# Earlier weight loads and splits, and half as many clears of twice the size, in a hashed-attention and MoE kernel

## The chip, the cores and the metric

The kernel runs on one core of one Trainium2 chip. The metric is the device time of one execution in microseconds. Before the change it is 832.31 us, the median of three runs (830.89 to 832.5).

## The reference

The inputs are q, k, v of shape (2, 8, 768, 64): 16 heads of 768 tokens. Each head's attention is masked by a hash: tokens attend to one another only if the signs of six projections agree. The result feeds a mixture of 8 experts (one expert per token, capacity 384), and that a dense layer pair.

```python
q_bits = (np.einsum('bhsd,dk->bhsk', q, proj) > 0)        # six bits, likewise for k
mask = q_bucket[:, :, :, None] == k_bucket[:, :, None, :]
scores = np.where(mask, scale * np.matmul(q, k.transpose(0, 1, 3, 2)), -1e9)
attn = softmax(scores);  x = attn @ v                      # rows of (1536, 512)
disp[e, counts[e]] = x[i]        # expert e = argmax of x @ w_gate, at most 384 rows each
y = relu(disp @ w1) @ w2;  out[i] = gate_w[i] * y[e, pos[i]]
h = out @ w_in;  result = (h * clip(h + 3, 0, 6) / 6) @ w_out
```

All products are made in two parts: a number is split into a high part, rounded to the matmul's format, and a low part, the rest. That holds for the weights too, hence the splits of weights spoken of below.

## The kernel before

The program has one instruction stream for each engine, written out by hand, with waits on semaphores between them. An engine takes its instructions in order. It has three stages: attention over the 16 heads (to about 325 us), routing and the 8 experts (to about 550 us), and the dense pair.

A head is named (turn, side), number 2*turn+side; tiles that alternate between heads have one copy a side. `LAST` is (7, 1). While TensorE works on head h, it also prepares h.next() (transposes of q and k at L1168, hash products at L1177) and multiplies the probabilities of h.prev() by v (L1246 to L1248).

One head in its steps, and where they stand:
- SP loads q and k (`load_qk`, L372) and v (`load_v`, L380) from memory.
- TensorE turns q and k; ScalarE writes the high part to q_ext (`high_qk`, L709), VectorE the low part to qk_lo (`low_qk`, L900).
- SP moves halves of these tiles between partitions by DMA (`place_head`, whose five moves are all at L384): k_ext<-q_ext, k_pair<-q_ext, k_pair<-qk_lo, then qk_lo<-q_ext, then k_ext<-q_ext (the hash bits). The first waits for `high_qk`. The fourth waits until the third has landed.
- VectorE makes the hash bits from the hash product (`bits`, L906). `bits` waits for the first two moves to have landed, since it writes over the same tile.
- TensorE makes the scores a first time, tile by tile (`max_tile`, L1191), VectorE takes their row maxima (`take_max`, L911, six a head) and negates them (`minus_max`, L916 to L919). In VectorE's order of a head, the `bits` of the next head stand between the fourth and the fifth `take_max`.
- TensorE turns the maxima (`turn_max`, L1205), ScalarE copies them (L713), and TensorE makes the scores a second time, as `cross` (L1220) and `direct` (L1228); ScalarE takes the exponential of each of the six tiles (L720) and its high part (L724), VectorE and GpSimd take low parts (L937, L614).

Beside the heads, three kinds of work for the expert stage are spread over the attention stage:
- The weights of expert 0, 4 MB in four loads (`load_part`, L406): two go out between `place_head(0,1)` and `load_v(1,0)`, two between `place_head(1,0)` and `load_v(1,1)`. ScalarE waits for all four before head (1,0), and then takes the high part of one eighth of them (`high_parts`, L734) in every head (turn, 0) from turn 1 on, with two in a row before `LAST`. GpSimd takes the low parts (`first_low`, L604) in heads (turn, 1), one before its work on `LAST`, one after it.
- The clears: the buffers x_slots and y_rows in memory are set to a row of zeros, in `CLEARS` = 12 pieces, each two DMAs (L430, L432), one piece a head, between `place_head(h)` and the `load_v` of the next. Before it scatters rows, GpSimd waits for `32 * CLEARS` on the clears' semaphore.
- At the end of the stage the first loads for expert 1 follow.

All loads, moves and clears of this stage are issued from SP, on one queue of the 16 DMA engines.

Of the kernel before, what the change touches and what calls it, by code (L numbers as in the profile page):

```python
# [19 lines left out]
def hashed_attention_moe_kernel(nc, q, k, v, proj, w_gate, w1, w2, w_in, w_out, out, capacity):  # L20
    B, H, S, D = q.shape
    NBITS = proj.shape[1]
    HEADS = B * H
# [37 lines left out]
    LOADS = 4  # L61
    LC = WC // LOADS
    CHUNKS = 8
    CC = WC // CHUNKS
    HB = 4
    CLEARS = HEADS - 4
    assert SLOTS // P % CLEARS == 0 and NT % CLEARS == 0
    assert WC == DC * F2 == FC2 * DM and ST > MT
    GT = BANK
# [19 lines left out]
    with ctx:  # L89
# [128 lines left out]
        def sem(name):  # L218
            return ctx.enter_context(nc.semaphore(name))
# [56 lines left out]
        raw_in = [sem(f"raw_in{i}") for i in range(LOADS)]  # L276
# [66 lines left out]
        def lo_use(h, first=False):  # L343

            return h.i * 3 + (1 if first else 0)

        def hash_use(h, first=False):

            return lo_use(h, first) + 1

        LAST = Head((HEADS - 1) // 2, 1)
# [11 lines left out]
        def _(sp):  # L363
# [3 lines left out]
            def load_qk(h, first=False):  # L367
                if not first:

                    sp.wait_ge(prep_full, h.i * 3 - 5)  # L370
                for part, source in enumerate((q_v, k_v)):
                    sp.dma_start(qk_raw[:, h.side, :, part * D:part * D + D],  # L372
                                 source[h.i, :, :].rearrange("p (c d) -> p c d", d=D)).then_inc(qk_in[h.side], 16)

            def load_v(h, first=False):
                if not first:

                    sp.wait_ge(v_lo_done, h.i - 1)
                    sp.wait_ge(v_summed, h.i - 1)
                sp.dma_start(v_raw[:, h.side, :, :].rearrange("p c d -> p (c d)"), v_v[h.i, :, :]).then_inc(v_in[h.side], 16)  # L380

            def move(to, of):

                return sp.dma_start(to.bitcast(F32), of.bitcast(F32))  # L384

            def place_head(h, first=False):
                sp.wait_ge(qk_hi_done, h.i + 1)
                move(k_ext[h.side][0:D, :], q_ext[h.side][D:2 * D, :]).then_inc(k_hi_placed, 16)
                move(k_pair[h.side][0:D, :], q_ext[h.side][D:2 * D, :]).then_inc(k_hi_placed, 16)

                sp.wait_ge(prep_free, lo_use(h, first))
                move(k_pair[h.side][D:2 * D, :], qk_lo[h.side][D:2 * D, :]).then_inc(k_lo_placed, 16)

                sp.wait_ge(prep_full, hash_use(h, first))
                sp.wait_ge(k_lo_placed, h.i * 16 + 16)
                move(qk_lo[h.side][D:2 * D, :], q_ext[h.side][0:D, :]).then_inc(q_hi_placed, 16)

                sp.wait_ge(prep_free, hash_use(h, first))
                move(k_ext[h.side][XR:XR + HB_ROWS, :], q_ext[h.side][XR + HB_ROWS:XR + 2 * HB_ROWS, :]).then_inc(k_bits_placed, 16)
# [5 lines left out]
            def load_part(side, s, source, arrived):  # L405
                sp.dma_start(w_raw[side][:, s * LC:(s + 1) * LC].rearrange("p (j n) -> p j n", n=source.shape[2]),  # L406
                             source).then_inc(arrived, 16)

            def of_expert(e, s):
                if s < DC // j1:  # L410
                    return w1_v[e, :, j1 * s:j1 * (s + 1), :]
                s -= DC // j1
                return w2_v[e, :, j2 * s:j2 * (s + 1), :]

            for side in range(2):
                load_qk(Head(0, side), first=True)
                load_v(Head(0, side), first=True)
            place_head(Head(0, 0), first=True)

            def next_head(h, between):  # L420
                load_qk(h.next())
                place_head(h)
                between()
                load_v(h.next())

            slots_pieces = x_slots.rearrange("(n r p) c -> n p r c", p=P, n=CLEARS)
            rows_pieces = y_rows.rearrange("(n r p) c -> n p r c", p=P, n=CLEARS)

            def clear_piece(n):
                sp.dma_start(slots_pieces[n, :, :, :],  # L430
                             zrow[:, :].unsqueeze(1).to_broadcast([P, SLOTS // P // CLEARS, XC])).then_inc(zero_out, 16)
                sp.dma_start(rows_pieces[n, :, :, :],  # L432
                             zrow[:, 0:DM].unsqueeze(1).to_broadcast([P, NT // CLEARS, DM])).then_inc(zero_out, 16)

            def first_weights(half):
                for s in range(half * LOADS // 2, (half + 1) * LOADS // 2):
                    load_part(0, s, of_expert(0, s), raw_in[s])

            next_head(Head(0, 1), between=lambda: first_weights(0))
            next_head(Head(1, 0), between=lambda: first_weights(1))  # L440
            sp.wait_ge(zrow_set, 1)
            with sp.Fori(1, HEADS // 2 - 1) as turn:
                for h in (Head(turn, 1), Head(turn + 1, 0)):
                    next_head(h, between=lambda: clear_piece(h.i - 3))
            place_head(LAST)

            def load_slots(e, side):
# [85 lines left out]
        def _(pool):  # L533
# [22 lines left out]
            first = Head(0, 0)  # L556
# [43 lines left out]
            def first_low(c):  # L600

                pool.wait_ge(whi_done, c + 1)
                cols = bass.ds(c * CC, CC)
                g.tensor_tensor(w_lo[0][:, cols], w_raw[0][:, cols], w_hi[0][:, cols].bitcast(F32),  # L604
                                ALU.subtract).then_inc(first_lo, 1)

            def low_v(h):
                pool.wait_ge(v_hi_done, h.i + 1)
                g.tensor_tensor(v_lo[:, h.side, :, :], v_raw[:, h.side, :, :], v_hi[:, h.side, :, 0:D].bitcast(F32),
                                ALU.subtract).then_inc(v_lo_done, 1)  # L610

            def low_probs(h, kc):
                pool.wait_ge(hi_done_a, h.i * BY_AP + (kc - BY_V + 1))
                g.tensor_tensor(probs_lo[:, kc, :], probs[:, kc, :], probs_hi[:, kc, :].bitcast(F32),  # L614
                                ALU.subtract).then_inc(lo_done_p, 1)

            def head(h, first=False, second=False, last=False, spare=None):
                if spare:
                    spare()
                if not first:  # L620
                    for kc in range(BY_V, C):
                        low_probs(h.prev(), kc)
                low_v(h)
                if not first and not second:
                    blend_mean(h.prev().prev())
                sum_v(h, first, second)

            head(first, first=True)
            head(first.next(), second=True)
            head(Head(1, 0))  # L630
            with pool.Fori(1, HEADS // 2 - 1) as turn:
                head(Head(turn, 1), spare=lambda: first_low(turn - 1))
                head(Head(turn + 1, 0))
            head(LAST, last=True, spare=lambda: first_low(CHUNKS - 2))
            first_low(CHUNKS - 1)
            low_probs(LAST, BY_V)
            low_probs(LAST, C - 1)
# [6 lines left out]

            pool.wait_ge(zero_out, 32 * CLEARS)
            pool.wait_ge(r_number, NT)
# [52 lines left out]
        def _(act):  # L699
# [31 lines left out]
            def high_parts(side, c):  # L731

                cols = bass.ds(c * CC, CC)
                a.activation(w_hi[side][:, cols], w_raw[side][:, cols], ACT.Copy).then_inc(whi_done, 1)  # L734
# [5 lines left out]
            def head(h, first=False, last=False, spare=None):  # L740
                for kc in range(BY_V, C):
                    if not first:
                        high_probs(h.prev(), kc)
                    if kc == BY_V and not last:
                        high_qk(h.next())
                if spare:
                    spare()
                if not first:
                    copy_out(h.prev())
                copy_max(h, last)  # L750
                for c in range(C):
                    exps(h, c, first)

            first = Head(0, 0)
# [5 lines left out]
            a.activation(back[D:D + 1, :, D:XW], zeros[D:D + 1, :].rearrange("p (h e) -> p h e", e=E),  # L760
                         ACT.Copy).then_inc(setup_a, 1)
            head(first, first=True)
            head(first.next())
            for s in range(LOADS):
                act.wait_ge(raw_in[s], 16)
            with act.Fori(1, HEADS // 2 - 1) as turn:
                head(Head(turn, 0), spare=lambda: high_parts(0, turn - 1))
                head(Head(turn, 1))
            head(LAST.prev(), spare=lambda: high_parts(0, CHUNKS - 2))
            high_parts(0, CHUNKS - 1)  # L770
            head(LAST, last=True)
            for kc in range(BY_V, C):
# [713 lines left out]
```

## Time and profile before

| | |
|---|---|
| median of 3 runs | 832.31 us |
| profiled execution, its own time | 832.5 us |
| its span, first to last instruction | 830.8 us |
| TensorE matmuls busy | 756.5 us (91%) |
| VectorE busy | 446.2 us (54%) |
| ScalarE busy | 356.7 us (43%) |
| GpSimd busy | 232.1 us (28%) |

Busy time is summed over the whole execution; in the profile PE is TensorE's matmuls, PEld its weight loads, DVE VectorE, ACT ScalarE, POOL GpSimd, and SPq the queue of instructions by which SP issues DMAs. "L384" is line 384 of the kernel. The chain of waits that ended last follows the execution backwards, from the last instruction to what released it, and so on: 79% of it lies on TensorE, 5% each on ScalarE, VectorE and DMA.

### The profile page before, as it was taken

Reading aid. Unit: us, or ns where it says so; the run is one execution under the profiler, and the core shown is the slowest. Engines: PE = TensorE matmul, PEld = TensorE weight load, DVE = VectorE, ACT = ScalarE, POOL = GpSimd, SP = SyncE. Lnnn points to the kernel's source line nnn. Section 1 sums busy time; section 2 is a strip of 40 time slices with the busy share of each in tenths; the row PEclk is TensorE's granted clock in tenths of the full one; section 3 lists DMA queues with packets and bytes.
Section 4 is the critical chain, followed back from the end, with each engine's and each line's share of the span. In section 5 each row is a group of like instructions: output and inputs, shape, how many; then the busy total and the mean of one; then the engine's idle time right before and its main releaser. Section 6 shows DMA issues by size and latency. Waiting matters only on the chain.

```text
span 830.8 us, 11762 instructions
## 1 busy us (share of the span) xinstructions
PE 756.5 (91%) x4117; PEld 618.6 (74%) x4117; DVE 446.2 (54%) x698; ACT 356.7 (43%) x543; POOL 232.1 (28%) x237
## 2 busy tenths in 40 slices
PE   3899999999999995089999999949999999999998
PEld 2677777777777763079999999938888888888886
DVE  4578777877778678345556665524344222322221
ACT  2454555555554553035555566514233322332223
POOL 3157676566767674501111010100000000000000
PEclk9999999999999998579999999979999999999999
DMA  5674544444545202456555665444001100010001
GB/s 120 175 196 114 145 125 118 126 111 109 133 116 145 66 1 101 154 176 243 200 217 205 239 213 178 187 152 169 1 1 50 51 1 1 0 52 1 1 0 51
DMA packets 62736, 92.25 MB, mean 111 GB/s; under 512 B 29935, under 2 KB 31983, under 8 KB 62192
## 3 DMA queue, kind: packets, MB, share of 16 engines
q1 hardware_dynamic: 59408, 85.50, 33.4%
q0 software_dynamic: 2240, 6.30, 2.1%
q8 instruction: 19, 0.31, 0.2%
q10 hardware_dynamic: 1056, 0.03, 0.1%
q14 instruction: 13, 0.11, 0.0%
HBM read 58.76 MB, written 19.94 MB: 95 GB/s over the span
## 4 chain that ended last, share of the span: by engine, by line
PE 79%; ACT 5%; DVE 5%; DMA 5%; issue 3%; POOL 2%; SPq 1%; ACTq 0%; POOLq 0%; DVEq 0%
PE score_ps L1352 11%; PE score_ps L1354 11%; PE score_ps L1353 11%; PE out_pair L1353 7%; PE out_pair L1354 7%; PE out_pair L1352 7%; PE score_ps L1191 3%; PE out_pair L1246 3%; ACT probs L720 3%; PE out_pair L1248 3%; PE out_pair L1247 3%; PE score_ps L1220 2%; PE out_pair L1261 2%; PE prep_ps L1177 2%; PE score_ps L1228 2%
## 5 line engine op out<-in xcount | busy, mean ns | idle before, releaser
L614 POOL TENSOR_TENSOR probs_lo<-probs,probs_hi 128x768 fp32r<-128x768 f32 x62 | 113.4, 1852 | 103.1 <-ACT probs_hi L724 103.1
L1352 PE MATMUL score_ps<-w_hi,h_hi 128*128 128x512 f32 x320 | 126.2, 394 | 0.4 <-DVE h_lo L1140 0.4
L1354 PE MATMUL score_ps<-w_hi,h_lo 128*128 128x512 f32 x320 | 124.7, 390 | 0.0
L1353 PE MATMUL score_ps<-w_lo,h_hi 128*128 128x512 f32 x320 | 124.6, 389 | 0.0
L1352 PE MATMUL out_pair<-xT_hi,w_hi 128*128 128x512 f32 (+1 forms) x320 | 112.1, 350 | 0.0
L1133 DVE SCALAR_TENSOR_TENSOR gated<-tclip,out_pair 128x512 f32<-128x512 f32 x48 | 33.0, 688 | 145.2 <-ACT tclip L835 145.2
L1354 PE MATMUL out_pair<-xT_hi,w_lo 128*128 128x512 f32 (+1 forms) x320 | 110.9, 347 | 0.0
L1353 PE MATMUL out_pair<-xT_lo,w_hi 128*128 128x512 f32 (+1 forms) x320 | 110.8, 346 | 0.0
L911 DVE TENSOR_REDUCE rowmax<-score_ps 128x1 f32<-128x768 f32 x96 | 88.7, 952 | 19.8 <-PE score_ps L1191 19.3
L835 ACT ACTIVATE tclip<-out_pair,three 128x512 f32<-128x512 f32 x48 | 33.2, 692 | 146.3 <-PE out_pair L1354 146.3
L1078 DVE TENSOR_TENSOR w_lo<-w_raw,w_hi 128x1024 fp32r<-128x1024 f32 x72 | 85.9, 1223 | 18.6 <-ACT w_hi L734 18.3
L734 ACT ACTIVATE w_hi<-w_raw 128x1024 fp32r<-128x1024 f32 (+1 forms) x80 | 81.6, 1054 | 0.0
L1246 PE MATMUL out_pair<-probs_hi,v_hi 128*65 128x512 f32 x192 | 66.6, 347 | 4.4 <-POOL probs_lo L614 3.4
L1352 PEld LDWEIGHTS score_ps<-w_hi,h_hi 128*128 128x128 f32 x320 | 60.1, 188 | 13.1 <-DVE h_lo L1140 1.2
L1354 PEld LDWEIGHTS score_ps<-w_hi,h_lo 128*128 128x128 f32 x320 | 60.1, 188 | 12.7
L1353 PEld LDWEIGHTS score_ps<-w_lo,h_hi 128*128 128x128 f32 x320 | 60.2, 188 | 11.9
L1352 PEld LDWEIGHTS out_pair<-xT_hi,w_hi 128*128 128x128 f32 x320 | 60.6, 189 | 7.5
L1353 PEld LDWEIGHTS out_pair<-xT_lo,w_hi 128*128 128x128 f32 x320 | 60.5, 189 | 7.4
L1354 PEld LDWEIGHTS out_pair<-xT_hi,w_lo 128*128 128x128 f32 x320 | 60.5, 189 | 7.5
L1248 PE MATMUL out_pair<-probs_lo,v_hi 128*65 128x512 f32 x192 | 64.8, 337 | 0.0
L1247 PE MATMUL out_pair<-probs_hi,v_lo 128*64 128x512 f32 x192 | 64.4, 335 | 0.0
L720 ACT ACTIVATE probs<-score_ps 128x768 f32<-128x768 f32 x64 | 48.9, 823 | 29.3 <-PE score_ps L1228 29.3
(150 smaller groups left out, 1301.6 us busy)
## 6 DMA issues: line engine op xcount, KB each, us to landing
w_raw<-in_moe_w SPq DMA_DIRECT2D x32, 1024.0 KB, 7.1
x_slots<-zrow SPq DMA_DIRECT2D x12, 513.0 KB, 4.3
rows_in<-x_slots SPq DMA_DIRECT2D x8, 513.0 KB, 8.8
w_raw<-in_moe_w_in SPq DMA_DIRECT2D x4, 1024.0 KB, 6.8
w_raw<-in_moe_w_out SPq DMA_DIRECT2D x4, 1024.0 KB, 12.4
qk_raw<-in_q SPq DMA_DIRECT2D x16, 192.0 KB, 3.3
qk_raw<-in_k SPq DMA_DIRECT2D x16, 192.0 KB, 3.4
v_raw<-in_v SPq DMA_DIRECT2D x16, 192.0 KB, 2.4
```

The costliest lines, as they stand in the source:

```text
L614: g.tensor_tensor(probs_lo[:, kc, :], probs[:, kc, :], probs_hi[:, kc, :].bitcast(F32), ALU.subtract).then_inc(lo_done_p, 1)
L720: a.activation(probs[:, c, :], exp_ps[c][:, 0:S], ACT.Exp, scale=SCALE).then_inc(exp_done, 1)
L734: a.activation(w_hi[side][:, cols], w_raw[side][:, cols], ACT.Copy).then_inc(whi_done, 1)
L835: a.activation(tclip[:, s % 2, :], g_ps[s % 2], ACT.Relu, bias=three[:, :]).then_inc(g_clip, 1)
L911: v.reduce_max(rowmax[:, h.side, c:c + 1], score_ps[c % 2][:, 0:S], AX.X).then_inc(max_taken, 1)
L1078: return v.tensor_tensor(w_lo[side][:, cols], w_raw[side][:, cols], w_hi[side][:, cols].bitcast(F32), ALU.subtract)
L1246: mm(out_pair[0:D + 1, lo:hi], v_h, probs_hi[:, kc, lo:hi], start=(kc == 0), stop=False)
L1247: mm(out_pair[0:D, lo:hi], v_l, probs_hi[:, kc, lo:hi], start=False, stop=False)
L1248: ins = mm(out_pair[0:D + 1, lo:hi], v_h, probs_lo[:, kc, lo:hi], start=False, stop=(kc == C - 1))
L1352: mm(out_tile, lhs[0], rhs[0], start=first, stop=False)
L1353: mm(out_tile, lhs[0], rhs[1], start=False, stop=False)
L1354: return mm(out_tile, lhs[1], rhs[0], start=False, stop=last)
```

## The change

`CLEARS` goes from 12 to 6, so each piece has twice the rows. A piece is issued once a turn, after all of `next_head(Head(turn, 1))`, that is behind `load_v`, no more in the middle of each `next_head`. The four weight loads of expert 0 are issued together, right behind `place_head(0,0)` and ahead of everything of head (1,0) and of the moves of (0,1). ScalarE waits for them before head (0,1), and takes high parts 0 to 6 in heads (0,1) to (6,1); the eighth stays ahead of `LAST`. GpSimd takes low parts 0 to 6 in heads (1,0) to (7,0), and the eighth, as before, behind its work on `LAST`.

```diff
--- before.py
+++ after.py
@@ -63,7 +63,7 @@
     CHUNKS = 8
     CC = WC // CHUNKS
     HB = 4
-    CLEARS = HEADS - 4
+    CLEARS = HEADS // 2 - 2
     assert SLOTS // P % CLEARS == 0 and NT % CLEARS == 0
     assert WC == DC * F2 == FC2 * DM and ST > MT
     GT = BANK
@@ -416,11 +416,12 @@
                 load_qk(Head(0, side), first=True)
                 load_v(Head(0, side), first=True)
             place_head(Head(0, 0), first=True)
-
-            def next_head(h, between):
+            for s in range(LOADS):
+                load_part(0, s, of_expert(0, s), raw_in[s])
+
+            def next_head(h):
                 load_qk(h.next())
                 place_head(h)
-                between()
                 load_v(h.next())
 
             slots_pieces = x_slots.rearrange("(n r p) c -> n p r c", p=P, n=CLEARS)
@@ -432,16 +433,13 @@
                 sp.dma_start(rows_pieces[n, :, :, :],
                              zrow[:, 0:DM].unsqueeze(1).to_broadcast([P, NT // CLEARS, DM])).then_inc(zero_out, 16)
 
-            def first_weights(half):
-                for s in range(half * LOADS // 2, (half + 1) * LOADS // 2):
-                    load_part(0, s, of_expert(0, s), raw_in[s])
-
-            next_head(Head(0, 1), between=lambda: first_weights(0))
-            next_head(Head(1, 0), between=lambda: first_weights(1))
+            next_head(Head(0, 1))
+            next_head(Head(1, 0))
             sp.wait_ge(zrow_set, 1)
             with sp.Fori(1, HEADS // 2 - 1) as turn:
-                for h in (Head(turn, 1), Head(turn + 1, 0)):
-                    next_head(h, between=lambda: clear_piece(h.i - 3))
+                next_head(Head(turn, 1))
+                clear_piece(turn - 1)
+                next_head(Head(turn + 1, 0))
             place_head(LAST)
 
             def load_slots(e, side):
@@ -627,11 +625,11 @@
 
             head(first, first=True)
             head(first.next(), second=True)
-            head(Head(1, 0))
+            head(Head(1, 0), spare=lambda: first_low(0))
             with pool.Fori(1, HEADS // 2 - 1) as turn:
-                head(Head(turn, 1), spare=lambda: first_low(turn - 1))
-                head(Head(turn + 1, 0))
-            head(LAST, last=True, spare=lambda: first_low(CHUNKS - 2))
+                head(Head(turn, 1))
+                head(Head(turn + 1, 0), spare=lambda: first_low(turn))
+            head(LAST, last=True)
             first_low(CHUNKS - 1)
             low_probs(LAST, BY_V)
             low_probs(LAST, C - 1)
@@ -760,13 +758,11 @@
             a.activation(back[D:D + 1, :, D:XW], zeros[D:D + 1, :].rearrange("p (h e) -> p h e", e=E),
                          ACT.Copy).then_inc(setup_a, 1)
             head(first, first=True)
-            head(first.next())
             for s in range(LOADS):
                 act.wait_ge(raw_in[s], 16)
-            with act.Fori(1, HEADS // 2 - 1) as turn:
-                head(Head(turn, 0), spare=lambda: high_parts(0, turn - 1))
-                head(Head(turn, 1))
-            head(LAST.prev(), spare=lambda: high_parts(0, CHUNKS - 2))
+            with act.Fori(0, HEADS // 2 - 1) as turn:
+                head(Head(turn, 1), spare=lambda: high_parts(0, turn))
+                head(Head(turn + 1, 0))
             high_parts(0, CHUNKS - 1)
             head(LAST, last=True)
             for kc in range(BY_V, C):
```

## Rows read from the trace of the kernel before

**Rows 1.** The chain of waits from 0 to 110 us: start us, length us, what
```profile
25.35 1.07 DVE q_ext L906
...
29.00 0.81 PE prep_ps L1205 x6
...
47.47 9.24 DMA w_raw<-in_moe_w
...
57.01 0.86 ACT probs_hi L724
```

**Rows 2.** SP's own issues in order of time: start us, length us, what
```profile
14.75 0.61 SPq L372 DMA_DIRECT2D qk_raw<-in_q  x1
...
21.04 0.60 SPq L384 DMA_DIRECT2D k_pair<-q_ext  x1
...
27.05 1.13 SPq L406 DMA_DIRECT2D w_raw<-in_moe_w  x2
...
28.27 0.41 SPq L380 DMA_DIRECT2D v_raw<-in_v  x1
...
29.39 0.75 SPq L372 DMA_DIRECT2D qk_raw<-in_k  x1
...
46.83 1.21 SPq L406 DMA_DIRECT2D w_raw<-in_moe_w  x2
...
58.64 0.53 SPq L384 DMA_DIRECT2D k_ext<-q_ext  x1
...
64.82 0.43 SPq L430 DMA_DIRECT2D x_slots<-zrow  x1
...
69.67 0.38 SPq L380 DMA_DIRECT2D v_raw<-in_v  x1
...
77.41 0.52 SPq L384 DMA_DIRECT2D k_ext<-q_ext  x1
...
280.29 0.49 SPq L384 DMA_DIRECT2D k_ext<-q_ext  x1
```

**Rows 3.** Last number: us from issue to landing; stretches at 20, 28, 64 us
```profile
k_pair<-q_ext SPq DMA_DIRECT2D x1, 192.0 KB, 3.0
...
v_raw<-in_v SPq DMA_DIRECT2D x1, 192.0 KB, 7.1
...
qk_raw<-in_k SPq DMA_DIRECT2D x1, 192.0 KB, 7.6
...
x_slots<-zrow SPq DMA_DIRECT2D x1, 513.0 KB, 4.2
...
y_rows<-zrow SPq DMA_DIRECT2D x1, 256.0 KB, 3.9
```

**Rows 4.** Line 406, issue to landing: the second load at 27 us, both at 47
```profile
DMA to landing us min/median/max: 7.1/7.1/7.1
...
DMA to landing us min/median/max: 6.2/7.7/9.2
```

**Rows 5.** Busy by engine PE, PEld, DVE, ACT, POOL; then clock, DMA share, GB/s
```profile
30.00:33.00 3.00, 2.86 (x9) 2.06 (x9) 0.42 (x1) 1.90 (x3) 0.00 (x0) 1.00 1.02 411
```

**Rows 6.** VectorE in order of time, with its wait in brackets
```profile
24.36 0.96 DVE L911 TENSOR_REDUCE rowmax<-score_ps 128x1 f32<-128x768 f32 x1 [2.05 <-PE score_ps L1191]
...
81.09 1.07 DVE L906 TENSOR_SCALAR q_ext<-prep_ps,above,weight 64x768 fp32r<-64x768 f32 x1
```

**Rows 7.** TensorE in order of time: two matmuls of one tile each row
```profile
34.70 0.84 PE L1220 MATMUL score_ps<-qk_lo,k_pair 128*128 128x512 f32 x2
...
35.91 0.51 PE L1220 MATMUL prep_ps<-qk_lo,k_pair 128*128 128x512 f32 x2
```

**Rows 8.** ScalarE and GpSimd in order of time, idle before in brackets
```profile
48.13 0.81 ACT L728 ACTIVATE out_T<-out_pair 65x768 f32<-65x768 f32 x1 [5.78 <-PE out_pair L1255]
...
57.93 7.28 POOL L614 TENSOR_TENSOR probs_lo<-probs,probs_hi 128x768 fp32r<-128x768 f32 x4 [9.25 <-ACT probs_hi L724]
...
297.93 7.24 POOL L614 TENSOR_TENSOR probs_lo<-probs,probs_hi 128x768 fp32r<-128x768 f32 x4 [4.65 <-ACT probs_hi L724]
```

## Prediction

> **What bounds the kernel now.** I read the page's chain first: TensorE holds 79% of it, so a change to the loads pays or costs only where TensorE waits for them. Then the chain of the first 110 us [rows 1]. There the reader is to see that the opening heads are not yet paced by TensorE: the chain runs through VectorE's `bits` (L906) at 25.35 us, into `turn_max` (L1205) at 29.00, and later through a weight load that lands at 56.7 and a ScalarE instruction at 57.01 that waited for it. Third, the SP queue in order of time [rows 2]: one moment repeats once a head, the first move of `place_head` (k_ext<-q_ext). From 77.41 to 280.29 there are eleven periods of 18.44 us each (none differs by more than 0.03), TensorE-paced; from 58.64 to 77.41 is 18.77, the one long period. So the stretch up to 57 us is where this change can act, besides what the doubled clears do to the steady period.
>
> **The weight loads, moved ahead of two heads' moves.** Now SP issues two 1 MB loads at 27.05 and two at 46.83, each pair behind the five moves of a head [rows 2]. After the change all four stand behind `place_head(0,0)`, where SP is now issuing qk_raw at 14.75. They are passed in front of: q and k of head (1,0), the five moves of head (0,1), v of (1,0), q and k of (1,1). What the profile shows on such passing: v_raw was issued at 28.27 behind the first pair and took 7.1 us, qk_raw's k at 29.39 took 7.6, while an unobstructed k_pair move takes 3.0 [rows 2, 3]. Landing times 35.4 and 37.0 both fall behind the second weight load, issued about 27.7 with 7.1 to land, so 34.8 [rows 4]. I read this as one queue served in order of issue, in which small transfers behind 2 MB wait for all of it, and then need 0.8 us each (37.0 less 35.4, over two).
>
> When do four loads end? The first two take what the pair at 27.05 took: 34.8 less 27.05, 7.75 us. Each further MB takes at least 1.05 MB at 411 GB/s, 2.55 us [rows 5], and at most what the second of the pair at 46.83 added: it was issued at 47.47 [rows 1] and took 9.2, landing at 56.7; the first landed at 46.83+6.2 = 53.0, so 3.7 us. The four end between 14.75+7.75+5.1 = 27.6 and 29.9; I take 3.1 a load, 28.7, between the two rows. Behind them come q and k of (1,0), then k_ext and k_pair of (0,1): four small ones at 0.8, 31.9 (bounds 30.0, at 0.6 each, and 33.3, at 0.85). Before, k_pair was issued at 21.04 and had landed by 24.0.
>
> SP's own time is hidden: two loads take 1.13 us to issue, four 2.3, q and k 1.4, so SP is free at 18.5, ahead of 20.5, the earliest for a move of (0,1), which waits for ScalarE (its k_pair is the one at 21.04).
>
> Who waits: VectorE takes its instructions in order, and `bits` of (0,1) waits for k_ext and k_pair to land. It stood at 25.35, right behind the row maximum at 24.36+0.96 [rows 1, 6]. Queued behind it on VectorE are the last two row maxima of head (0,0) and `minus_max`, and for that waits `turn_max` on TensorE, then ScalarE's `copy_max` and all six exponentials. None of it has other work to cover it: TensorE has only the first `cross` left, 1 us. So the whole shift passes on: 31.9 less 25.35 is 6.5 us later (bounds 4.6 and 8.0). The later moves of (0,1) (low parts, q high parts, bits) come 0.8 us apart and land at about 35.9; TensorE needs them only when it ends head (0,0), some 8 us after `turn_max`, so they cost nothing more. v of (1,0) and q, k of (1,1) find the queue empty.
>
> **ScalarE's wait for the loads** moves from the start of head (1,0) to that of (0,1), at 37.6 before and 44 after; the loads are in by 29.9, so it costs nothing. Its old place goes: that ScalarE began at 57.01 only when the load had landed, GpSimd's low parts behind it, TensorE behind these. What it was worth is the long period less the steady one, 18.77-18.44 = 0.3 us gained. The bound above is the 0.9 us of the wait itself, below 0. Next late there is TensorE itself, so no more comes out.
>
> **The splits.** The eight high parts (ScalarE, about 1.05 us) come one head earlier, except the last; the low parts (GpSimd, 2.4 us) too. None is added. In head (0,1) the high part falls into 5.78 us in which ScalarE sat idle, the first low part into GpSimd's idle 9.25 us [rows 8]; the eleven steady periods alternate between heads with a split and heads without, and are alike to 0.03 us [rows 2]. I cost them at 0; uncovered, one would cost its own 1 or 2.4 us. In the last head GpSimd loses one low part ahead of its probs_lo, but it had idled 4.65 us for ScalarE there [rows 8]: 0. The last high part stays where it is.
>
> **The clears.** Twelve pairs become six of twice the size, moved from ahead of `load_v` to behind it. SP issues twelve DMAs fewer, at 0.4 us each, in time that it spends waiting: 0. The bytes are the same. The new pair is issued behind v_raw at 69.67, so at about 70.1, followed by q and k and then by the moves of the next head at 77.41. The present pair, issued from 64.82, lands 3.9 us after an issue at 65.4: 4.5 us for 0.79 MB [rows 2, 3]. Twice the bytes take 4.5+0.79/0.411 = 6.4 us at least, 9.0 at most; the queue is free of the pair at 76.5 to 79.1 and of q and k at 78.1 to 80.7. The moves' data needs 1.6 us more to k_pair's landing, so 79.7 to 82.3 against 77.98+3.0 = 81.0 before, and `bits` starts at 81.09 [rows 3, 6]. A loss of 0 to 1.2 us a clear. I take 0: the fixed part of a landing is paid once.
>
> **Clock.** The granted clock in 30 to 33 us is given as 1.00 [rows 5], but the matmuls say otherwise: the pair at 34.70 takes 0.84 us, that at 35.91 takes 0.51 [rows 7]; the first stands at the lower level (1.2 GHz), the second at 2.4, after TensorE had been busy without long gaps since 29.0. If it rises as long after the new start, nothing changes but the shift. The 4.6 us between 30.7 and 35.3 would shrink by the ratio 0.51/0.84 to 2.8, so an earlier rise gives back up to 1.8 us; a later one could cost as much. I take 0. The Trainium skill (TensorE: Matmul & The Clock Gate, Part 1) says the clock is raised by sustained activity and that the point varies from run to run; by it the sum would lie anywhere within these same 1.8 us.
>
> **Sum.** +6.5 - 0.3 = +6.2 us on the profiled execution, whose own time is 832.5: 838.7. The median of the runs is 0.2 below that execution: 838.5.
>
> **Rivals.**
> A. The moves overtake. If small transfers are not held up by the big ones, k_pair lands as before, `bits` starts at 25.35, and only the gain of 0.3 is left: 832.0, no change that a measurement can tell (0.2%, 1.7 us, is about what one can). This is the other side: not slower. It decides on when k_pair of (0,1) lands, before or after 25.3. For it: that qk_raw at 29.39 took 7.6 could be its own narrow rows beside a busy engine. Against: both landed behind the weights, in order of issue, v_raw too, which has wide rows. The Trainium skill (DMA: Bandwidth & Descriptors, Queues, rings and completion order) states that completion is not first-in first-out for an issuing engine, since a later DMA can finish its data before an earlier one does. The trace agrees with the page's other half alone, that descriptors are taken in order; by a free overtaking the sum would be 832.0.
> B. The clears hold up the moves. Place: heads (2,0), (3,0) and so on, six times, price up to 1.2 us each, from the point where pair, q and k together need over 8.3 us from 70.1. With the 6.2 that makes up to 838.5+7 = 845.7. For it: the landing of k_pair and the start of `bits` lie 0.1 us apart, so there is no slack. Against: the drain time with a shared fixed part leaves 1.3 us.
> C. TensorE's clock rises early in the longer first head: 838.5-1.8 = 836.7.
>
> **Chances.** Forecast 0.78 (its own range 834.5 to 842: the delay's 4.6 to 8.0 less 0.3, with 1.8 us of clock to either side cut to what is likely together, and 1 us of scatter), A 0.08, B 0.08, C 0.06. The range takes in C and part of B: 834.5 to 843; outside are A and most of B. Faster: 0.03, half of A's scatter; same 0.06; slower 0.91.
>
> **What would show it.** Right: in the changed kernel the four weight issues stand at 15 to 17 us, L906 of (0,1) starts at about 32 with a wait for k_pair, the L1205 that stood at 29.0 stands at 35.5, and the period stays 18.44. Wrong: L906 of (0,1) at 25.4 (then A); periods alternating between 18.44 and more (then B); any head behind 60 us whose distance from its old place differs from 6.2 by more than 1 us.

## The result, and the profile after

The changed kernel takes 876.33 us, the median of four runs (875.14 to 880.29), against 831.95 before: a ratio of 1.0543, 95% interval [1.0508, 1.058]. It is 44 us slower, where 6 us slower was forecast. Its profiled execution is a lighter one, 867.35 us, so the trace shows 35 of the 44 us; the mean granted clock of the four timed executions is lower still (0.934 to 0.942 against 0.949 in the trace), of which more below.

From the page of the changed kernel, the span, the busy times, and the chain of waits by engine:

```profile
span 865.4 us, 11757 instructions
...
PE 775.1 (90%) x4117; PEld 635.6 (73%) x4117; DVE 433.7 (50%) x698; ACT 358.1 (41%) x543; POOL 231.7 (27%) x237
...
PE 77%; DMA 8%; DVE 6%; ACT 4%; issue 3%; SPq 2%; POOL 1%; DVEq 0%; POOLq 0%; ACTq 0%
```

TensorE's matmuls take 19 us more busy time than before for the same 4117 instructions, and DMA's part of the chain rose from 5% to 8%. ScalarE and GpSimd are about as busy as before (358.1 and 231.7 us); VectorE is 12.5 us less busy, which I did not follow up. So there are two new things: time spent waiting for transfers, and matmuls that run slower.

SP's issues in order of time (start, length), which answer to [rows 2]:

```profile
14.91 2.72 SPq L406 DMA_DIRECT2D w_raw<-in_moe_w  x4
17.67 2.53 SPq L372 DMA_DIRECT2D qk_raw<-in_q  x1
20.24 3.66 SPq L372 DMA_DIRECT2D qk_raw<-in_k  x1
23.95 2.59 SPq L384 DMA_DIRECT2D k_ext<-q_ext  x1
26.58 0.63 SPq L384 DMA_DIRECT2D k_pair<-q_ext  x1
...
47.48 0.51 SPq L384 DMA_DIRECT2D k_ext<-q_ext  x1
...
77.20 0.42 SPq L431 DMA_DIRECT2D x_slots<-zrow  x1
77.81 0.38 SPq L433 DMA_DIRECT2D y_rows<-zrow  x1
...
84.36 0.52 SPq L384 DMA_DIRECT2D k_ext<-q_ext  x1
...
106.02 0.53 SPq L384 DMA_DIRECT2D k_ext<-q_ext  x1
```

The first move of head (1,0), at 40.18 before, stands at 47.48: 7.3 us late. From 84.36 to 106.02 it is 21.66 us instead of 18.44. The periods alternate: every second one is 18.4 to 18.5, the six between are 21.66, 25.00, 23.18, 23.18, 24.24 and 22.64. Together these six are 29.3 us over the steady period. With 7.3 for the first head, less 0.3 for the long period that is gone, that is the 36.3 us by which the first move of `LAST` comes later (316.55 against 280.29). The whole span is longer by 34.6 us, so 1.7 us come back behind the attention stage; where, I did not trace.

Landing times (last number, us) of k_pair of head (0,1), of the doubled pair at 77 us, and of k_pair behind it; then VectorE's `bits` (now L902) of (0,1) and of (2,0); they answer to [rows 3] and [rows 6]:

```profile
k_pair<-q_ext SPq DMA_DIRECT2D x1, 192.0 KB, 6.0
...
x_slots<-zrow SPq DMA_DIRECT2D x1, 1026.0 KB, 9.2
...
y_rows<-zrow SPq DMA_DIRECT2D x1, 512.0 KB, 9.1
...
k_pair<-q_ext SPq DMA_DIRECT2D x1, 192.0 KB, 5.8
```

```profile
32.69 1.07 DVE L902 TENSOR_SCALAR q_ext<-prep_ps,above,weight 64x768 fp32r<-64x768 f32 x1 [7.22 <-DMA k_pair<-q_ext]
...
90.75 1.07 DVE L902 TENSOR_SCALAR q_ext<-prep_ps,above,weight 64x768 fp32r<-64x768 f32 x1 [2.77 <-DMA k_pair<-q_ext]
```

The y part of the pair was issued at 77.81 and landed at 86.9, 9.7 us after the pair's first issue; the single pair took 4.5. k_pair of the next head, issued at 84.92, took 5.8 us instead of 3.0, and `bits` waited 2.77 us for it. In the trace `bits` waits at each of the six clears, 2.1 to 3.4 us, 16.3 in all.

TensorE after that wait, in order of time (idle before in brackets), and then stretches of the changed kernel as in [rows 5] (busy of PE, PEld, DVE, ACT, POOL; granted clock; DMA share; GB/s):

```profile
92.86 0.62 PE L1216 MATMUL score_ps<-qk_lo,k_pair 128*128 128x512 f32 x2 [0.56 <-DVE rowmax L907]
94.79 0.52 PE L1201 MATMUL prep_ps<-identr,negmax_hl 128*2 128x128 f32 x6 [1.31 <-DVE negmax_hl L915]
```

```profile
79.00:80.00 1.00, 1.00 (x7) 0.85 (x7) 0.99 (x2) 1.00 (x3) 0.00 (x0) 1.00 1.09 394
80.00:81.00 1.00, 1.00 (x7) 0.67 (x5) 0.97 (x2) 1.00 (x3) 0.00 (x0) 1.00 1.41 84
81.00:82.00 1.00, 1.00 (x6) 0.69 (x5) 1.00 (x2) 1.00 (x3) 0.00 (x0) 1.00 0.82 53
82.00:83.00 1.00, 1.00 (x10) 0.82 (x8) 1.00 (x2) 0.55 (x1) 0.38 (x1) 1.00 0.86 96
...
134.00:136.00 2.00, 0.93 (x9) 0.70 (x7) 1.08 (x5) 0.00 (x0) 1.84 (x4) 0.82 0.14 46
136.00:138.00 2.00, 2.00 (x10) 1.90 (x10) 0.00 (x0) 0.80 (x1) 1.47 (x1) 0.50 0.44 107
...
144.00:146.00 2.00, 2.00 (x9) 1.69 (x8) 0.78 (x1) 1.42 (x2) 0.00 (x0) 0.62 0.00 0
146.00:148.00 2.00, 2.00 (x15) 1.64 (x14) 1.42 (x2) 1.75 (x3) 0.15 (x1) 1.00 0.00 0
```

At 92.86 and 94.79 TensorE had stood still for 0.56 and 1.31 us, behind `take_max` and `minus_max`, as the prediction's chain has it. The first four stretches show the drain of the pair, that is how its bytes leave the queue: 394 GB/s, and then, with the DMA engines about as busy (shares of 0.82 to 1.41), 84, 53 and 96. The last four show the clear that follows: after the idle time from 132 to 135 us the granted clock falls to 0.50, the lower level (1.2 GHz), and stays there until 145, while TensorE is busy without a gap. That head took 25.0 us. Such a fall follows each of the six waits, for 3 to 10 us.

### The profile page after: what moved, and what is told of

It is laid out like the page before. It is cut to its first block, busy times and chain, and to the rows that moved or that the text cites. A ratio compares the mean times of both kernels' runs of the same rounds, so it can differ in the third digit from the quotient of the medians.

```text
span 865.4 us, 11757 instructions
## 1 busy us (share of the span) xinstructions
PE 775.1 (90%) x4117; PEld 635.6 (73%) x4117; DVE 433.7 (50%) x698; ACT 358.1 (41%) x543; POOL 231.7 (27%) x237
## 2 busy tenths in 40 slices
DMA packets 62543, 92.24 MB, mean 107 GB/s; under 512 B 29743, under 2 KB 31791, under 8 KB 62000
## 4 chain that ended last, share of the span: by engine, by line
PE 77%; DMA 8%; DVE 6%; ACT 4%; issue 3%; SPq 2%; POOL 1%; DVEq 0%; POOLq 0%; ACTq 0%
PE score_ps L1348 10%; PE score_ps L1350 10%; PE score_ps L1349 10%; PE out_pair L1348 7%; PE out_pair L1350 7%; PE out_pair L1349 7%; DMA k_pair<-q_ext 5%; PE score_ps L1224 3%; PE score_ps L1216 3%; PE out_pair L1257 3%; PE score_ps L1187 3%; PE out_pair L1242 2%; PE out_pair L1244 2%; PE out_pair L1243 2%; PE prep_ps L1337 2%
```

## Experiments

Differences are against the kernel before, timed side by side with each kernel; its median was 829.4 to 831.8 us. L902 and L384 are as above.

**One part at a time.** Clears as before, all else changed:

```diff
-    CLEARS = HEADS // 2 - 2
+    CLEARS = HEADS - 4
@@ next_head, and the loop on SP
                 place_head(h)
+                between()          # clear_piece(h.i - 3) for both heads of a turn
                 load_v(h.next())
-                clear_piece(turn - 1)
```

> The changed kernel with the clears as before (12 pairs, between place_head and load_v). Theory: the loss is two losses, 7.3 us where the moves of head (0,1) stand behind 4 MB of weights, once, and 3.2 to 6.6 us at each of the six doubled clears; with the clears back only the first is left: 839 us (838 to 842), all periods from the second head on 18.44. Rival 1, the earlier splits lengthen the heads: still above 860. Rival 2, an early stall leaves TensorE's clock worse for the whole stage: still above 850, with periods over 18.6.

Measured 840.62 against 831.81, ratio 1.0103 [1.0088, 1.0119]. All periods from the second on are 18.42 to 18.46. `bits` of (0,1) waited 8.65 us, L1201 (`turn_max`) stood at 37.61 instead of 29.00. Both rivals fall: 8.8 us belong to the weights, the rest of the 44 to the clears.

Only the clears changed:

```diff
-    CLEARS = HEADS - 4
+    CLEARS = HEADS // 2 - 2
-                for h in (Head(turn, 1), Head(turn + 1, 0)):
-                    next_head(h, between=lambda: clear_piece(h.i - 3))
+                next_head(Head(turn, 1), between=lambda: None)
+                clear_piece(turn - 1)
+                next_head(Head(turn + 1, 0), between=lambda: None)
```

> The kernel before with only the clears of the change (six doubled pairs behind load_v). Theory: 832 plus the loss of the clears alone, 44 less 7: 869 us (860 to 875), six periods of 21.6 us or more. Rival 1, splits: 832. Rival 2, the loss needs the early weights: below 845.

Measured 864.48 against 831.81, ratio 1.0402 [1.0383, 1.042], six periods of 22.6 to 24.6 us. 32.7 and 8.8 make 41.5 of the 44; the rest is no more than the runs with falling clocks scatter (859 to 866 us here).

Only the splits changed:

```diff
+            for s in range(LOADS // 2):
+                act.wait_ge(raw_in[s], 16)
+            head(first.next(), spare=lambda: high_parts(0, 0))
+            head(Head(1, 0))
             for s in range(LOADS // 2, LOADS):
                 act.wait_ge(raw_in[s], 16)
@@ then as in the change, on ScalarE and on GpSimd
```

> The kernel before with only the splits one head earlier; ScalarE waits for the first two loads before head (0,1), for the other two before the loop. Theory: 832 (831.2 to 832.8), the splits lie in idle time. Rival 1: above 850, up to the whole loss.

Measured 831.33 against 831.81, ratio 0.9995 [0.9985, 1.0005]. The long period is gone; SP's first moves of (1,1) and (2,0), 58.64 and 77.41 before [rows 2], here:

```profile
58.78 0.53 SPq L384 DMA_DIRECT2D k_ext<-q_ext  x1
...
77.23 0.52 SPq L384 DMA_DIRECT2D k_ext<-q_ext  x1
```

18.45 us. So the splits cost nothing, and the 0.3 us are there in the trace, too little for the runs to tell.

**Size or place of the clears.** Twelve single pairs in the late place, and six doubled pairs in the early place:

```diff
 # first kernel: CLEARS = HEADS - 4, and
+                for h in (Head(turn, 1), Head(turn + 1, 0)):
+                    next_head(h)
+                    clear_piece(h.i - 3)
 # second kernel: CLEARS as changed, and
+                next_head(Head(turn, 1), between=lambda: clear_piece(turn - 1))
+                next_head(Head(turn + 1, 0))
```

> The changed kernel with 12 single-size pairs, each behind load_v, so the late place with half the size, twelve times. Theory, drain time decides: a single pair is out of the queue 4.5 to 5 us after its issue, q and k 1.7 us later, before the moves start some 7 us after the pair, so bits wait little: 839 to 846 us. Rival, the place behind load_v costs by itself whatever the size: each of 12 heads loses, 860 or more.

> The changed kernel with the six doubled pairs put between place_head and load_v of head (turn, 1), some 5.5 us earlier than behind load_v. Theory: the pair must be out of the queue when the next head's moves are issued; issued 13 us ahead of them and needing about 10, it is: 840 us (838 to 843), all periods 18.44, as with single pairs. Rival: doubled pairs cost by their size wherever they stand (bandwidth, landing): 860 or more.

Measured 840.89 against 831.81 (1.0117 [1.0101, 1.0132]) for single pairs late, 839.26 against 830.68 (1.0096 [1.0079, 1.0113]) for doubled pairs early. Both have all periods at 18.42 to 18.50: neither size nor place costs, only both together. The single pair in the late place lands so (last number, us):

```profile
x_slots<-zrow SPq DMA_DIRECT2D x1, 513.0 KB, 4.8
...
y_rows<-zrow SPq DMA_DIRECT2D x1, 256.0 KB, 4.7
```

4.7 after an issue at 77.3, by 82.0; q and k follow, and the moves at 84 find the queue empty. The doubled pair takes 9.1 to 9.2 us in the late and in the early place: twice the bytes take about twice the time.

**What makes the doubled pair slow.** Four kernels, all otherwise as changed. The first clears only 2048 of the 2052 bytes of each row of x_slots, and the number column by a DMA of its own; the second reads from a zero tile of full width; the third also writes each partition's rows side by side; the fourth does only the latter.

```diff
 # first
-                sp.dma_start(slots_pieces[n, :, :, :], zrow[:, :]...to_broadcast([P, SLOTS // P // CLEARS, XC]))
+                sp.dma_start(slots_pieces[n, :, :, 0:DM], zrow[:, 0:DM]...to_broadcast([P, SLOTS // P // CLEARS, DM]))
 # second and third
-        zrow = at("zrow", [P, XC], F32)
+        zrow = at("zrow", [P, 4, XC], F32)      # no to_broadcast in clear_piece
 # third and fourth, for x_slots and y_rows
-            slots_pieces = x_slots.rearrange("(n r p) c -> n p r c", p=P, n=CLEARS)
+            slots_pieces = x_slots.rearrange("(n p r) c -> n p r c", p=P, n=CLEARS)
```

> The changed kernel, but the pieces of x_slots clear only the 512 data columns (rows of 2048 bytes instead of 2052); the one number column of all rows is set by a DMA of its own at the end of the attention stage. Theory A, the slow part of the drain (DMA engines busy at 50 to 100 GB/s from 80 to 83 us of the changed kernel) is the 4 bytes by which a row exceeds 2048: the pair lands in about 6.4 us, bits waits little, 841 to 848. Theory B, the drain is slow through the bytes alone: within 1% of 876. The single column DMA may itself cost some us at the end.

> The changed kernel, its clears read from a zero tile of the full width (4 rows a partition) instead of one row read four times. Theory A, the drain of a doubled pair (9.7 us against 4.5 of a single one) is slow on the writing side, the memory: the pair still lands 9 us after its issue, 870 to 880. Theory B, it is slow because each DMA engine reads one and the same row again and again: the pair lands in under 7 us and the time falls below 855.

> The kernel with the zero tile of full width, and each partition now writes its rows of a piece side by side in memory (8208 and 4096 bytes in a stretch instead of 2052 and 2048). Theory A, the slow middle of the drain is the number of short rows that must be written: the pair lands in under 7 us, bits waits under 1 us, 838 to 846. Theory B, it is the bytes written to memory in one go, whatever their rows: the pair lands in 7.4 to 8.8 us as with the tile alone, 855 to 865.

> The changed kernel with only the order in memory changed (rows of a partition side by side), the source again one row read over and over. Theory A as for the other run: under 850 if the writing rows decide. Theory B: 870 to 880, landing 9 us. If the source decides together with the rows: in between, near the 860 of the tile alone.

| | us (before) | ratio, 95% interval |
|---|---|---|
| rows of 2048 bytes | 869.0 (830.68) | 1.0423 [1.0362, 1.0484] |
| whole zero tile | 860.08 (829.74) | 1.0377 [1.0342, 1.0412] |
| whole tile, rows side by side | 837.87 (829.38) | 1.0105 [1.0088, 1.0122] |
| rows side by side alone | 865.9 (829.38) | 1.0447 [1.0429, 1.0465] |

The landing of the y part of the first doubled pair, in the second, third and fourth kernel, and two stretches of the third:

```profile
y_rows<-zrow SPq DMA_DIRECT2D x1, 512.0 KB, 8.8
```

```profile
y_rows<-zrow SPq DMA_DIRECT2D x1, 512.0 KB, 6.2
```

```profile
y_rows<-zrow SPq DMA_DIRECT2D x1, 512.0 KB, 9.5
```

```profile
80.00:81.00 1.00, 1.00 (x8) 0.86 (x7) 1.00 (x2) 1.00 (x2) 0.00 (x0) 1.00 1.07 451
81.00:82.00 1.00, 1.00 (x7) 0.56 (x5) 0.97 (x2) 1.00 (x3) 0.00 (x0) 1.00 0.87 353
```

The 4 bytes are not the cause: with rows of 2048 bytes the y part still took 8.8 us and 38 us were lost, so theory A of the first falls. The whole tile took a part of the loss away: 30.3 us against 44.4 for the changed kernel, which was not timed beside it, and 36.5 for the fourth kernel. The waits of `bits` fell to between 0.7 and 2.7 us, and in the two heads where it was about 1 us or less, no time was lost. So neither theory of the second stands. The third removes the clears' loss: its pair lands in 6.2 us, at 451 and 353 GB/s where the changed kernel had 84 and 53, and all periods are 18.42 to 18.48. It has 2304 DMA packets fewer (60239 against 62543). The fourth has as many packets as the changed kernel, its y part took 9.5 us, and most of the loss is there.

So the slow drain goes only when the rows are long at both ends: as long as the source is one row read again and again, rows side by side in memory leave the number of packets as it was. That is a remedy more than a cause. The number of packets is not all of it, since the whole tile alone has as many (62542) and lost less. Nor are packets of 2 KB slow as such. The first row below is the changed kernel from 24 to 25 us, reading weights; the second is its slow stretch, from 80 to 83 us:

```profile
DMA packets 201, 0.41 MB, mean 406 GB/s; under 512 B 3, under 2 KB 3, under 8 KB 201
```

```profile
DMA packets 114, 0.23 MB, mean 78 GB/s; under 512 B 0, under 2 KB 0, under 8 KB 114
```

Both are packets of 2 KB on average. The second row also rules out that the narrow rows of the q and k loads, issued right behind the pair, make the slow stretch: no packet in it is under 2 KB. It is not the moment either: in the early place the pair has it too, 57 and 62 GB/s from 75 to 77 us, about as long after its issue. Why this write runs well for about 0.8 MB (394 GB/s at its best) and at under 100 GB/s for the next three microseconds stays open.

**The queue or the DMA engines.** The same clears from ScalarE's queue; and the weights from ScalarE's queue, with the clears as before:

```diff
 # first: in ScalarE's head(), for heads (turn + 1, 0)
                 copy_max(h, last)
+                clear_piece(act, turn)
                 for c in range(C):
 # second: on ScalarE, ahead of head(first); not on SP
+            for s in range(LOADS):
+                act.dma_start(w_raw[0][:, s * LC:(s + 1) * LC]..., of_expert(0, s)).then_inc(raw_in[s], 16)
```

> The changed kernel with the six doubled pairs issued from ScalarE's queue, ahead of its exponentials, 1 to 2 us before the place on SP. Theory, order of the queue: q, k and the moves no longer stand behind the pair, and k_pair lands within 4 us of its issue: 841 to 850. Rival, the DMA engines' time: the same engines are busy, and the loss stays above 865.

> Clears as before, splits and ScalarE's wait as in the change, the four weight loads issued at about 10 to 13 us from ScalarE's queue instead of at 15 us from SP's. Theory, order in one queue: the moves of (0,1) stand behind nothing on SP's queue and share the DMA engines with the weights, so k_pair lands 1 to 3 us late instead of 8.6: 832 to 836 us. Rival, the DMA engines' time is what is short: at least 838. Where bits waits little and the 18.77 period is gone, the gain of 0.3 us may show.

The first measured 845.8 against 830.68 (1.0192 [1.016, 1.0223]), its profiled execution 839.59, the three others 844.6 to 849.65. The time is as the theory has it and far from its rival's 865, but the trace does not bear out the theory's reason: v_raw, issued on SP's queue while the pair was on ScalarE's, took 8.6 us instead of 2.4, and `bits` of (2,0) still waited:

```profile
89.40 1.07 DVE L905 TENSOR_SCALAR q_ext<-prep_ps,above,weight 64x768 fp32r<-64x768 f32 x1 [1.30 <-DMA k_pair<-q_ext]
```

The pair was issued 2.1 us earlier than on SP, and 1.30 us of waiting costs only 0.1 us of the period. That explains the gain without the queue, though this run changed both and cannot tell them apart. The second kernel speaks against the queue as well: 840.41 against 829.74, ratio 1.0119 [1.0104, 1.0134], no better than on SP's queue. ScalarE issued the loads already at 8.3 us, ahead of the moves of head (0,0), and the chain of that kernel shows what the moves cost, though no more stood ahead of them on their own queue than before:

```profile
10.34 9.95 DMA k_pair<-qk_lo
...
20.87 6.76 DMA k_ext<-q_ext
```

Before, these two (192 and 96 KB) took 3.2 and 2.5 us. My theory that order in one queue holds the small transfers up falls as a sole cause: beside loads on a second queue they were held up about as long. The run is not a clean contrast, since the loads came earlier than I meant.

**The clock.** Twelve repeats of the small matmul of `turn_mean` in every head (turn, 1), which keep TensorE busy while `bits` waits; and the same in the kernel before:

```diff
                 pe.wait_ge(v_summed, h.i + 1)
+                for _ in range(fill):      # 12 for side 1, else 0
+                    mm(mean_T_ps, v_sum[:, h.side, :], mean_w[:, :], start=True, stop=True)
```

> The changed kernel with 12 extra small matmuls (turn_mean repeated) in each head (turn, 1), which fill the time in which TensorE waits for VectorE at a doubled clear. The waits of bits stay. Theory, part of each clear's price is TensorE's clock, which falls to the lower level after the wait and stays there for 3 to 9 us: filled, the clock holds and 8 to 15 us come back, 860 to 870 (2 us spent in head (0,1)). Rival, the price is the wait alone: 876 to 880.

> The kernel before with the 12 extra matmuls in each head (turn, 1), seven heads, to price them by themselves. Theory: they stand open in these heads and cost some 1.5 to 2.7 us each, 842 to 850 us, so that filling a gap at a doubled clear gives back more than the 19 us seen. Rival, they are hidden: 832 to 834.

Filled, the changed kernel takes 857.01 us against 830.68 (1.031 [1.0291, 1.0329]), 19 us less than unfilled, though it does more. The fill alone costs 849.36 against 829.74, 19.6 us, its periods 21.04 to 21.10. In the filled changed kernel four of the six heads at a clear take the very same 21.07 to 21.10: with the clock held, waits of 1.5 to 3.3 us vanish in the fill. In the other two of its trace, where `bits` waited longest (4.0 and 3.8 us), the clock fell all the same, and they took 27.54 and 25.79; that trace is of an execution of 868.63 us, the four others took 856.4 to 857.9. Against its own kernel before, the filled one loses 26.3 us, which is no more than the fill (19.6) and the weights (8.8) lose by themselves: of the 35.7 us that the clears cost in the changed kernel (876.3 less 840.6) nothing is left. The fill only puts other work where TensorE stood idle, so without the clock it could give no time back; the 19 us are the least that the clock costs. Two stretches of it behind a wait of 3.3 us, clock after the fifth pair of numbers:

```profile
94.00:96.00 2.00, 2.00 (x15) 1.53 (x14) 1.51 (x2) 0.00 (x0) 1.80 (x3) 1.00 0.01 5
...
100.00:102.00 2.00, 2.00 (x14) 1.76 (x14) 0.66 (x3) 0.29 (x1) 0.47 (x1) 1.00 0.57 141
```

**What is left when nothing is lost.** Splits early, doubled clears early, weights as before (the kernel with only the splits and the doubled pairs in the early place, joined):

> The parts of the change that cost nothing, together: splits one head earlier, six doubled clear pairs in the old place between place_head and load_v, weight loads as before. Theory: 831.4 (830.8 to 832), the 0.3 us of the long period gained, nothing lost. Rival, doubled pairs near the first weight loads or moves lose something: 833 or more.

829.83 against 829.74, ratio 1.0000 [0.9991, 1.001]. No version beat the kernel before.

## Why the prediction was wrong

**The weight loads: right in mechanism, somewhat under.** Forecast were 6.5 us (4.6 to 8.0). The last load landed at 28.9 (28.7 forecast) and k_pair at 32.6 (31.9), all in order of issue; the four small transfers behind the loads took 0.9 us each, where I had 0.8. L1201 stood at 36.35 against 29.00, 7.35 us late, in the changed kernel, and 8.6 in the kernel with only the clears put back, which is over my upper bound. SP's own time, which I had called hidden, was not: its issues behind the weights took 2.5, 3.7 and 2.6 us each, where they had taken 0.5 to 0.7, so k_pair went out at 26.58 instead of 21.04. That was still before the loads had ended, so whether it made k_pair land later is not shown. Rival A is dead, 32.6 against 25.3. But the loads' damage does not hang on the one queue, as I had read it: from ScalarE's queue they cost 10.7 us.

**ScalarE's wait and the splits: right**, 0.3 us gained in the trace, nothing lost.

**The clears: wrong, and this is the step that failed**, "I take 0: the fixed part of a landing is paid once". There is hardly a fixed part: 4.5 us became 9.7. My upper bound, twice the 4.5, was the measured value all but 0.7 us; I chose the lower one from 411 GB/s, a rate at which weights are read from memory in rows of 4 KB, for rows of 2 KB written to it. k_pair landed at 90.7 where its undisturbed landing would be 87.9 (84.92+3.0), so 2.8 late where the bounds said 0 to 1.2. Beside the 0.7 us of the drain, q, k and the moves behind it took 3.8 us instead of my 3.2. Rival B, with 0.08, named place and mechanism, and the periods alternate as it said; it priced them at a fifth to a quarter (7.2 us of 35.7, or of 29.3 in the trace). Its own condition has a slip: by the sum before it the pair, q and k had to need over 9.3 us from 70.1, not 8.3.

**The clock: priced at the wrong place.** I weighed it once, for the first head, at up to 1.8 us (2.0 by the 0.64 and 0.36 us at which the pairs follow one another), and there, in the trace of the changed kernel, it did nothing: the first move of head (1,0) is late by 7.3 us, as L1201 is. In rival B I did not price it at all. By the trace TensorE stood idle behind `take_max` and `minus_max` for 10.9 us at the six clears (eleven gaps like the two shown); the heads grew by 29.3; the other 18.4 fall into some 40 us spent at 1.2 GHz. In the timed runs there is more of it: of the clears' 35.7 us some 25 would be the clock's, an estimate that takes the idle time to be that of the trace. The Trainium skill (TensorE: Matmul & The Clock Gate, "HAM oscillation") tells of matmul bursts that wait for DMA and start at the low clock again each time. The rows agree that the clock is low again after a wait for DMA, each time; here it fell behind two short gaps (0.6 and 1.3 us in the rows shown), shorter than the waits of the page's example, and up to 3 us after the second.

**The slack.** I took `bits` to have none, as it starts 0.1 us after k_pair lands. By the traces it has about 1.2 us of slack: a wait of 1.30 us cost 0.1. My whole bound of 0 to 1.2 a clear would have cost nothing. The step from harmless to over 4 us lies between 1.30 and 1.95 us of waiting (the latter in the kernel with the whole zero tile, a period of 22.64).

## What to carry to other kernels

Before a transfer is made larger ahead of a small one that an in-order engine waits for, take its drain time from a row of the same direction and row length, and doubt any part of it that you call fixed: only with long rows at both ends did this one come near its forecast (6.8 us for 6.4). Price a new gap on TensorE twice, once for the wait and once for the clock behind it; here the second was the larger. Do not count on another queue to take a small transfer out of the way of a large one; here it did not.

## What the runs showed of the hardware

- A 1.5 MB write in rows of 2 KB from one repeated row landed after 9.7 us; in rows of 8 and 4 KB, from a tile as large, after 6.8; in rows of 2 KB from a tile as large, after 9.4. With only the order in memory changed its y part took 9.5.
- Moves between partitions of 192 and 96 KB took 3.2 and 2.5 us before, and 10 and 6.8 beside 4 MB of loads on another engine's queue.
